# Two fused networks behind an attention: the weighing of a unit placed behind the next unit's transposes

## The reference

```
scores = q @ k.T / sqrt(64), masked; a = softmax(scores); x = a @ v
h = x @ w_in  (512 -> 2048);  y = (h * sigmoid(1.702 h)) @ w_out
out = (sigmoid(y @ w_gate) * (y @ w_val)) @ w_out2      (512 -> 1536 -> 512)
```

## Time and profile before

| | us |
|---|---|
| median of 3 runs | 716.38 (715.59 to 716.92) |
| profiled execution, its own time | 715.4 |
| span of the profiled execution | 713.6 |
| busy PE | 687.4 (96%) |
| busy ACT | 397.4 (56%) |
| busy POOL | 354.7 (50%) |
| busy DVE | 278.1 (39%) |

### The profile page before, as it was taken

The page is one execution under the profiler, slowest core; times in us unless marked ns, Lnnn a source line. Parts: engine busy times, 40 slices in busy tenths (PEclk is TensorE's granted clock), DMA queues, the critical chain, the costliest instruction groups (busy, mean ns, idle before and its releaser), DMA issues.

```text
span 713.6 us, 10667 instructions
## 1 busy us (share of the span) xinstructions
PE 687.4 (96%) x3632; PEld 562.0 (79%) x3632; DVE 278.1 (39%) x820; ACT 397.4 (56%) x855; POOL 354.7 (50%) x419
## 2 busy tenths in 40 slices
PE   6777999999999999999999999999999999999998
PEld 5556788888788888788888788888878888788886
DVE  6888434344444333343443433333232222311112
ACT  4787466667665666466676666565444444433321
POOL 2574245555455545266565655464335445544530
PEclk9999999999999999999999999999999999999999
DMA  6322332343433223143325323311132233233001
GB/s 199 137 75 75 114 113 100 101 144 126 141 116 108 89 73 104 60 148 129 99 98 177 125 82 134 119 60 36 60 141 90 91 126 138 103 110 114 0 1 59
DMA packets 23798, 73.41 MB, mean 103 GB/s; under 512 B 3616, under 2 KB 3616, under 8 KB 23744
## 3 DMA queue, kind: packets, MB, share of 16 engines
q1 hardware_dynamic: 23744, 72.73, 30.9%
HBM read 69.57 MB, written 3.15 MB: 102 GB/s over the span
## 4 chain that ended last, share of the span: by engine, by line
PE 88%; ACT 4%; DVE 3%; issue 2%; SPq 1%; DMA 0%; ACTq 0%; DVEq 0%
PE ps L781 22%; PE ps L782 21%; PE ps L783 21%; PE ps L847 5%; PE ps L848 5%; PE ps L849 5%; PE ps L768 1%; PE ps L766 1%; PE ps L767 1%; PE ps L751 1%; PE ps L738 1%; PE ps L752 1%; PE ps L739 1%; ACT probs L434 1%; DVE probs_n L605 1%
## 5 line engine op out<-in xcount | busy, mean ns | idle before, releaser
L379 POOL TENSOR_TENSOR w_lo<-w_raw,w_hi 128x256 fp32r<-128x256 f32 (+1 forms) x336 | 277.4, 857 | 270.7 <-ACT w_hi L428 270.7
L781 PE MATMUL ps<-x_hi,w_hi 128*128 128x512 f32 x480 | 195.6, 407 | 1.2 <-issue 0.9
L782 PE MATMUL ps<-x_lo,w_hi 128*128 128x512 f32 x480 | 188.2, 392 | 0.0
L783 PE MATMUL ps<-x_hi,w_lo 128*128 128x512 f32 x480 | 187.6, 391 | 0.0
L428 ACT ACTIVATE w_hi<-w_raw 128x1024 fp32r<-128x1024 f32 (+1 forms) x84 | 104.3, 1242 | 42.5 <-PE ps L849 25.9
L621 DVE SCALAR_TENSOR_TENSOR ps<-squashed,ps 128x512 f32<-128x512 f32 x84 | 58.2, 692 | 151.2 <-PE ps L783 88.5
L452 ACT ACTIVATE g_hi<-ps 128x512 fp32r<-128x512 f32 x84 | 50.1, 597 | 110.9 <-DVE ps L621 110.9
L783 PEld LDWEIGHTS ps<-x_hi,w_lo 128*128 128x128 f32 x480 | 90.2, 188 | 20.0
L781 PEld LDWEIGHTS ps<-x_hi,w_hi 128*128 128x128 f32 x480 | 90.2, 188 | 15.8 <-issue 1.7
L782 PEld LDWEIGHTS ps<-x_lo,w_hi 128*128 128x128 f32 x480 | 90.6, 189 | 12.8
L626 DVE TENSOR_TENSOR g_lo<-ps,g_hi 128x512 fp32r<-128x512 f32 x84 | 58.0, 691 | 49.5 <-ACT g_hi L452 49.3
(11 more groups left out here) (75 smaller groups left out, 1006.3 us busy)
## 6 DMA issues: line engine op xcount, KB each, us to landing
w_raw<-in_w SPq DMA_DIRECT2D x36, 768.0 KB, 4.3
w_raw<-in_w SPq DMA_DIRECT2D x48, 512.0 KB, 3.3
q_raw<-in_q_t SPq DMA_DIRECT2D x48, 128.0 KB, 3.7
k_raw<-in_k_t SPq DMA_DIRECT2D x48, 128.0 KB, 3.6
v_raw<-in_v_t SPq DMA_DIRECT2D x12, 256.0 KB, 3.7
out_x<-out_sb SPq DMA_DIRECT2D x12, 256.0 KB, 2.2
v_sink_raw<-in_v_sink SPq DMA_DIRECT2D x2, 160.0 KB, 2.9
k_sink_raw<-in_k_sink SPq DMA_DIRECT2D x4, 8.0 KB, 2.2
```

The source lines that it names most:

```text
L379: pool.tensor_tensor(w_lo[:, slot, at:at + part], w_raw[:, slot, at:at + part], w_hi[:, slot, at:at + part].bitcast(F32), ALU.subtract).th ...
L781: pe.matmul(ps[:, bank, :], hi, act_hi, start=first, stop=False)
L782: pe.matmul(ps[:, bank, :], hi, act_lo, start=False, stop=False)
L783: return pe.matmul(ps[:, bank, :], lo, act_hi, start=False, stop=last)
```

## The change

Beside the networks the weighing moves from offset +1 to +3, where it follows the transposes directly (they stand first in `attention_at`). The copy of a finished group moves from +2 to +4, where it stands ahead of the PT work of the same slot. The wait of the last unit's transposes is another: its weighing neighbour no longer stands before it.

```diff
-OFF_SCORE, OFF_WEIGH, OFF_NORMALISE, OFF_TRANSPOSE = 0, 1, 2, 3
-OFF_SPLIT, OFF_X, OFF_PT = 1, 2, 4
+OFF_SCORE, OFF_NORMALISE, OFF_TRANSPOSE, OFF_WEIGH = 0, 2, 3, 3
+OFF_SPLIT, OFF_PT, OFF_X = 1, 4, 4
...
-                    pe.wait_ge(masked, u + 1 if u % CHUNK_UNITS == CHUNK_UNITS - 1 else u + 2)
+                    if u % CHUNK_UNITS == CHUNK_UNITS - 1:
+
+                        pe.wait_ge(pt_ready, u)
+                    else:
+                        pe.wait_ge(masked, u + 2)
```

## The result

The changed kernel took 722.61 us in the median of 6 runs (720.03 to 725.50), the kernel before 716.65 (715.59 to 718.15): a ratio of 1.0082, 95% interval 1.0055 to 1.0108. That is 4 to 8 us slower. The sign and the kind of waits were as forecast; the time lies 0.6 us outside the range, and the forecast of 719.9 is 2.7 us short.

What follows compares the result with a forecast made beforehand. PE's instruction stream was taken as the bound. Waits of +5.2 us, -1.2 at chunk boundaries and 0 for seams gave +4.0 on the profiled 715.4, or 719.4 (720.4 from the median); forecast 719.9, range 717.0 to 722.0.

Steps and rivals of the forecast that it cites:

- The move of X is the costly part: Scores behind slots 5, 9, 13, 17, 25 wait for `pt_lo`, queued behind the finished group's copy: +5.2 us in all.
- In chunk 0 `v_sinks(1)` gets ahead of `pt_lo` too, 1.15 us, wait 1.25: Slot 17, chunk 0: sinks' splitting on DVE delays `pt_lo` by 1.15 us, so the next score waits 1.25.
- None of the waits is longer than 1.3 us, and I add nothing for the clock: Beside the networks: PE's new waits are too short to lower its granted clock, so 0 us is added.
- The early loop is not touched: Early loop, before the networks' stretch: code unchanged, forecast difference 0 us.
- The seam at 0: 64 places where weighing joins the transposes: cost unchanged, 0; bounds 0.6 us loss to 6.4 us gain.
- What the move of X gives back, -1.2 us: Two chunk boundaries, slot 33: `g_lo` now precedes `x_lo`, so PE's 0.60 us wait goes, twice.
- Rivals 1 and 2: Seams: last transpose 0.05 us cheaper, net +0.8, chance 0.10; or 0.10 saved per seam, net -2.4, chance 0.05.
- rival 3: Slots 5, 9, 13, 17: the short waits of 0.25 and 0.15 us vanish, net +2.3, 718.2; chance 0.10.
- Rival 4: Delay cascades behind slots 5, 9, 13: late masks hold transposes, slot 29 or step 15 may miss; +1 to +3 us; chance 0.13.

Runs made afterwards that it cites:

- the kernel with X at +5: Changed kernel with PT work ahead of the group copy, sinks' splitting in slot 18, copy at +5 (slot 33: +4): 715.15 us, ratio 0.9964 to the kernel before.

## Why the prediction was wrong

*The move of X is the costly part*: right, in place and order. The sum from three distances gave 0.25, 0.15 and 1.15 us of wait, and the differences to the kernel before were 0.25, 0.16 and 1.05. Exchanging the two blocks took all of them away.

*In chunk 0 `v_sinks(1)` gets ahead of `pt_lo` too, 1.15 us, wait 1.25*: this step failed. The place was right and the size was not. I took the duration from a row in which POOL stood idle; POOL starts `w_lo` at 204.98 there, 0.3 us after the two instructions end. Behind `x_lo` they fall into `w_lo` and take 2.6 us: a wait of 2.80. That is 1.55 us of the miss of 2.7, and more than the 0.6 by which the time left the range. The runs that move the two in and out of POOL's work show it.

*None of the waits is longer than 1.3 us, and I add nothing for the clock*: failed with it. Behind the wait of 2.8 us PE's clock can be at its lower level (1.2 GHz) for some 3 us, worth 1.6 us. How often it does in the changed kernel as it stands is open: in the one trace of it, it did not.

*The early loop is not touched*: right for the code, but I set a profiled execution of 715.4 against a median of 716.38 without asking what lay between them. The early loop's clock does. It made 5 us of spread in one and the same kernel, and the changed kernel's profile had 1.5 us more of it than the one I summed against. The range had nothing for it. In the two traces this and the sinks' splitting make 3.0 us over the forecast of +4.0, and small terms take 0.4 of it back. At the same mean granted clock of 0.997, one run of the changed kernel had 720.03 and nine of the kernel before 715.40 to 715.64: 4.5 us.

*The seam at 0*: close. Less than 0.02 us a seam, about 1.0 us in all, in the changed kernel's favour. In its own trace most of it is hidden by what I left out on the other side: the second matmul of a score that has waited starts 0.20 instead of 0.12 us after the first, at ten places, 0.75 us together.

*What the move of X gives back, -1.2 us*: right, 0.60 twice.

Rivals 1 and 2 are out by the seam measured; rival 3 is out, the short waits are real. Rival 4 is out for this kernel: set beside the kernel with X at +5, whose PE does the same work in the same order, it loses time only at the ten scores that wait and their second matmuls, and nowhere at transposes or behind slots 21 and 29 (no step of 0.03 us or more). With PT ahead of X the meeting of mask and transposes is real, 0.2 us at six places.

## What to carry to other kernels

When work is put ahead of something in an engine's written order, add the distances of starts along the new chain up to the instruction that the bound engine waits for, and compare with the distance that it had; that came out to within 0.1 us here, in all places but the one where an instruction's duration had changed. Before using an instruction's duration at a new time, look at what the other engines do at that time, not at the old one. And of two blocks that share a place in the order, the one that feeds the bound engine goes first: here that alone turned 0.8% slower into no change, and with the sinks moved as well into 0.3% faster.

## What the runs showed of the hardware

- DVE instructions on SBUF alone took 0.84 to 1.20 us instead of 0.41 to 0.43 (80x512 cast) and 1.36 to 1.39 instead of 0.68 (16x512 subtraction) while POOL subtracted in SBUF. Those that read PSUM kept their 0.42.
- The granted clock fell to half for about 3 us behind PE waits of 2.8 and 3.4 us beside the networks, in one of two profiles with the wait of 2.8; behind the waits of 1.2 us and less there, it did so in no profile.
- In the early loop, whose longest waits are about 2 us and come every four units, the clock fell at times that differ from run to run. Two more idle matmuls per unit cost about 4.4 us on the best run, and took the spread from 5.7 to 0.6 us.
- A PE score of 260 columns that had waited for DVE was followed by its second matmul 0.20 us later, and one that had not waited 0.12 later.
